# The up projection of the second MLP: twelve column blocks against seven block products per unit, with the sum of stages parked in the output

## What is computed

```python
def reference(**kwargs):
    ...
    x = ...                       # retention over q, k, v: B=2, S=768, 8 heads of 64 -> x is (2, 768, 512)
    x = _moe_ref(x=x, **moe_kwargs)
    return _moe2_ref(x=x, **moe2_kwargs)

def _moe_ref(x, w_theta, w_tok_r, w_tok_i, w_ch):
    theta = x @ w_theta
    zr, zi = x * np.cos(theta), x * np.sin(theta)
    y = np.einsum('ts,bsd->btd', w_tok_r, zr) + np.einsum('ts,bsd->btd', w_tok_i, zi)
    u = x + y
    return u + np.maximum(u @ w_ch, 0.0)

def _moe2_ref(x, w_tok1, w_tok2, w_ch1, w_ch2):
    xt = x.transpose(0, 2, 1)
    h = np.maximum(xt @ w_tok1, 0.0) @ w_tok2          # 768 -> 256 -> 768 tokens
    u = x + h.transpose(0, 2, 1)
    h2 = np.maximum(u @ w_ch1, 0.0) @ w_ch2            # 512 -> 1536 -> 512 channels
    return u + h2
```

## Time and profile before

| what | value |
|---|---|
| time, median of 3 runs | 435.82 us (435.68 to 436.22) |
| the profiled execution: time, span of its instructions | 435.77 us, 434.0 us |
| PE busy, PE weight loads busy | 426.8 us, 388.3 us |
| DVE, ACT, POOL busy | 278.4, 158.3, 85.3 us |
| `tokens_down` on PE | from 228.24 to 244.91 us |
| up projection on PE | from 244.91 to 342.87 us |
| down projection on PE and its last sum | from 342.87 us to the end |

### The profile page before, as it was taken

How to read it: one execution, slowest core, us unless ns; L and a number is a source line. 1 busy time by engine, 2 the same in 40 slices (tenths; PEclk the granted TensorE clock), 3 DMA queues, 4 the chain that set the end, 5 groups by cost and what they waited for, 6 DMA issues and landing times.

```text
span 434.0 us, 6621 instructions
## 1 busy us (share of the span) xinstructions
PE 426.8 (98%) x2748; PEld 388.3 (89%) x2748; DVE 278.4 (64%) x383; ACT 158.3 (36%) x231; POOL 85.3 (20%) x75
## 2 busy tenths in 40 slices
PE   7999999999999999999999999999999999999997
PEld 4778878899999999999889988888888899999997
DVE  3799998799999995234415304525211599999951
ACT  1364564744455456112214311101202443555500
POOL 1322241000300006980005803303000110000000
PEclk9999999999999999999999999999999999999999
DMA  8975797540594102030000000003000468340121
GB/s 301 419 269 198 253 270 146 103 145 2 157 220 159 48 2 97 2 115 31 0 2 0 2 0 0 2 0 142 5 0 2 72 154 171 113 67 26 54 74 73
DMA packets 10478, 42.25 MB, mean 97 GB/s; under 512 B 1104, under 2 KB 3280, under 8 KB 8656
## 3 DMA queue, kind: packets, MB, share of 16 engines
q1 hardware_dynamic: 7344, 26.74, 16.6%
q0 software_dynamic: 2960, 14.94, 15.6%
q10 hardware_dynamic: 144, 0.14, 0.1%
HBM read 38.68 MB, written 3.15 MB: 96 GB/s over the span
## 4 chain that ended last, share of the span: by engine, by line
PE 96%; DVE 2%; DMA 1%; ACT 0%; issue 0%; ACTq 0%; DVEq 0%
PE ps L982 85%; PE ps L999 3%; PE ps L1039 3%; PE ps L1053 2%; PE ps L1130 1%; PE ps L1013 1%; PE ps L1029 1%; DMA qkv_in<-qkv 1%; DVE prob L712 1%; DVE h_ops_c L906 0%; DVE w_sq L696 0%; ACT h_ops_c L657 0%; DVE x_lo L736 0%; DVE res L731 0%; DVE res L942 0%
## 5 line engine op out<-in xcount | busy, mean ns | idle before, releaser
L982 PE MATMUL ps<-u,ch 128*128 128x512 f32 x432 | 98.1, 389 | 0.0
L982 PEld LDWEIGHTS ps<-u,ch 128*128 128x128 f32 x432 | 81.1, 188 | 16.8
L982 PE MATMUL ps<-tw,zs 128*128 128x384 f32 x504 | 88.1, 335 | 0.0
L982 PEld LDWEIGHTS ps<-tw,zs 128*128 128x128 f32 x504 | 87.3, 188 | 0.1
L982 PE MATMUL ps<-h_ops_c,w 128*128 128x384 f32 x312 | 57.0, 335 | 0.2
L982 PEld LDWEIGHTS ps<-h_ops_c,w 128*128 128x128 f32 x312 | 54.2, 188 | 0.8 <-DVE h_ops_c L906 0.8
L899 DVE SCALAR_TENSOR_TENSOR h_a<-ps,h_a 128x512 f32<-128x512 f32 (+1 forms) x16 | 8.9, 558 | 44.3 <-PE ps L982 26.3
L580 ACT ACTIVATE zs<-z 128x768 fp32r<-128x768 f32 x28 | 23.7, 846 | 37.0 <-PE ps L982 37.0
L982 PE MATMUL ps<-ut,w_sq 128*128 128x384 f32 x192 | 35.5, 338 | 0.0
L982 PEld LDWEIGHTS ps<-ut,w_sq 128*128 128x128 f32 x192 | 33.0, 188 | 0.0
L982 PE MATMUL ps<-w_sq,x_hi 128*128 128x512 f32 x96 | 30.7, 401 | 0.7 <-DVE w_sq L696 0.7
(11 more groups left out here) (106 smaller groups left out, 639.0 us busy)
## 6 DMA issues: line engine op xcount, KB each, us to landing
qkv_in<-qkv SPq DMA_DIRECT2D x11, 1024.0 KB, 7.5
raw<-tok POOLq DMA_DIRECT2D x7, 1152.0 KB, 9.0
stage<-weights SPq DMA_DIRECT2D x11, 512.0 KB, 3.4
w_raw<-ch POOLq DMA_DIRECT2D x7, 768.0 KB, 6.8
cols_out<-res SPq DMA_DIRECT2D x16, 192.0 KB, 1.8
raw<-tok SPq DMA_DIRECT2D x6, 384.0 KB, 8.6
w_raw<-ch SPq DMA_DIRECT2D x2, 768.0 KB, 5.3
raw<-tok POOLq DMA_DIRECT2D x3, 384.0 KB, 9.2
```

Of the source, the lines that this page charges most:

```text
L982: mm = pe.matmul(dst, left(l), right(r), start=first and n == 0, stop=last and n == 2, skip_group_check=True)
```

## The change

The up projection too becomes a 2 x 2 block product with seven block products. u of a sequence is cut into channel halves (rows) and token halves (columns); `w_ch1` into its input halves and, for each of six groups phi of 256 hidden channels, two output halves. A unit is (phi, sequence): `UNITS` has 12. Each unit has seven products of 2 k-blocks x 3 passes over 384 tokens, so 504 matmuls of 384 columns stand where 432 of 512 stood. Units go in pairs: product j of unit n, then product j of unit n + 1, then j + 1 (six pairs).

- Of each sequence the seven operands `u_op(b, o)` are made of four blocks and four sums (`sum_u`): seven copies on ACT (`u_high`), seven subtractions (`u_low`). DVE does the low parts of sequence 0 and two of sequence 1, POOL the five others. u_low of the whole u is gone.
- The first product is negated. Products 0, 2, 4 and 6 are added up in one bank (A); after 0, 2 and 4 the bank's running sum is copied or combined: ACT keeps it after products 0 and 2 (`keep_p1`, `keep_p6`) and keeps product 1 of bank B (`keep_p5`), DVE combines after 3, 4 and 5 (`add_p3`, `add_p7`, `add_p2`). A product that adds to a bank waits for the reader of what stood in it: product 2 for `keep_p1`, 3 for `keep_p5`, 4 for `keep_p6`, 6 for `add_p7`.
- POOL's `split_w1` makes, of each 1024-wide piece, 1792 columns of weights: three blocks plain and four with sums (four additions of 256 columns in place). Pieces 0 to 2 are split ahead of the stage, 3 and 4 after pair 1, 5 after pair 3. Stage buffers go from three to two.
- `res` is written to the output after `keep_u2` (2 transfers, "parked"), since its space is wanted for units, and read back into `total` in four transfers during the last pair; `keep_down` adds to `total`, one addition a cell.
- The order of the seven down products, their signs and the loads of `w_ch2` are others; the first load starts once the last piece of `w_ch1` is split, the second only when the whole up projection is done.

```diff
-NSTAGE = 3
+NSTAGE = 2
+UP = 7
+UP_W = (0, 6, 5, 4, 3, 1, 2)
+UP_BANK = (0, 1, 0, 1, 0, 2, 0)
+UP_FRESH = (0, 1, 5)
+UNITS = [(0, 0), (1, 0), (0, 1), (1, 1)] + [(phi, b) for phi in range(2, NPHI) for b in range(B)]
...
+BK_UP = (((1, 2), (4, 5)), ((3, 6), (3, 6)), ((7, 0), (7, 0)))
...
+            for b in range(B):
+                sp.wait_ge(u2_kept, 2 * NK * (b + 1))
+                sp.dma_start(out[b].rearrange("k p s -> p k s"), res[:, b, :, :]).then_inc(spilled[b], 16)
+            load_piece(N_PIECES - 1)
             split_done(sp, N_PIECES - 1)
-            for i in range(2):
-                sp.dma_start(w2_raw[:, i, :], ch2[i]).then_inc(w2_in[i], 16)
+            sp.dma_start(w2_raw(0), ch2[1]).then_inc(w2_in[0], 16)
...
+            sp.wait_ge(up_ready, up_count(len(UNITS) - 1, 3))
+            for b, r in ((0, 0), (1, 1), (1, 0), (0, 1)):
+                sp.dma_start(total[:, b, 2 * r:2 * r + 2, :],
+                             out[b, 2 * r:2 * r + 2].rearrange("k p s -> p k s")).then_inc(back[b][r], 16)
+            sp.wait_ge(up_ready, len(UNITS) * UP)
+            sp.dma_start(w2_raw(1), ch2[0]).then_inc(w2_in[1], 16)
...
+                    if part:
+                        pool.wait_ge(w1_lo, 2 * phi + 1)
+                        pool.tensor_tensor(a11, a11, a21, ALU.add).then_inc(w1_sum, 1)
...
+                        pool.tensor_tensor(a12, a12, a22, ALU.add).then_inc(w1_sum, 1)
...
+                    pool.tensor_scalar(home[:, 0, to], raw1[:, at], 1.0, 1.0, ALU.mult, ALU.mult).then_inc(w1_hi, 1)
...
+                    pool.wait_ge(w1_hi, 2 * phi + part + 1)
+                    pool.tensor_tensor(home[:, 1, to], raw1[:, at], f32(home[:, 0, to]),
+                                       ALU.subtract).then_inc(w1_lo, 1)
...
+            for o in U_PLAIN:
+                u_low(o)
...
             pool.wait_ge(w2_lo, 1)
-            add_w2(0, 2, s2_part)
+            pool.dma_start(w2_raw(0), ch2[3]).then_inc(s1_part, 16)
+            pool.wait_ge(s1_part, 16)
+            add_w2(0, 2, s1_w_in)
...
+            for pair in range(NPAIRS):
+                n = 2 * pair
+                last = pair == NPAIRS - 1
+                if pair == 0:
+                    u_high(0, 4)
+                keep_p1(n)
...
+                keep_p1(n + 1)
+                if pair == 0:
+                    u_high(0, 5)
+                    u_high(0, 6)
...
+                keep_p5(n)
+                keep_p5(n + 1)
...
+            for pair in range(NPAIRS):
+                if pair == 0:
+                    u_low(1, 0)
+                    sum_u(1, 0)
+                    sum_u(1, 1)
+                elif pair == 2:
+                    h_op_low(0, 0)
+                    h_op_low(0, 1)
...
+                add_p3(n)
+                add_p3(n + 1)
+                if pair == 0:
+                    u_low(1, 3)
+                    sum_u(1, 2)
+                for m in second:
+                    second_units(m, 0, 1)
+                add_p7(n)
+                add_p7(n + 1)
...
+                elif j == 2:
+                    pe.wait_ge(p1_kept, n + 1)
+                elif j == 3:
+                    pe.wait_ge(p5_kept, n + 1)
+                elif j == 4:
+                    pe.wait_ge(p6_kept, n + 1)
+                elif j == 6:
+                    pe.wait_ge(sum_22, n + 1)
+                for k in range(2):
+                    mm = three(up_bank(n, j), lambda l: w1_home(phi)[:, l, at:at + P],
+                               lambda r: u_op(b, j)[:, r, k * HS:(k + 1) * HS], j in UP_FRESH and k == 0, k == 1)
```

More of the change, by code:

```diff
@@ L23 @@
 PIECE = 1024
-NSTAGE = 3
+NSTAGE = 2
 NQ = 3
-TILES = 3
 NPHI = NF // 2
@@ new lines, in first_units @@
+            def first_units(n, row, half):
+                to = unit_block(n, row, half)
+                if (row, half) == (1, 0):
+                    act.wait_ge(up_ready, up_count(n, 6))
+                    act.activation(to, up_bank(n, 6), ACT.Relu).then_inc(first_21, 1)
+                else:
+                    added, kept = {(0, 1): (sum_12, first_12), (1, 1): (sum_22, first_22),
+                                   (0, 0): (sum_11, first_11)}[row, half]
+                    act.wait_ge(added, n + 1)
+                    act.activation(to, to, ACT.Relu).then_inc(kept, 1)
@@ new lines, in u_low @@
+            def u_low(b, o):
+                dve.wait_ge(u_hi[b], o + 1)
+                hi, lo, done = f32(u_part(b, o, 0)), u_part(b, o, 1), u_minus_lo if b else u_lo[0]
+                if o in U_MINUS:
+                    dve.scalar_tensor_tensor(out=lo, in0=u_raw(b, o), scalar=-1.0, in1=hi, op0=ALU.mult,
+                                             op1=ALU.subtract).then_inc(done, 1)
+                else:
+                    dve.tensor_tensor(lo, u_raw(b, o), hi, ALU.subtract).then_inc(done, 1)
@@ new lines, in _, with add_p3 @@
+            keep_u2(0, 0, 2)
+            sum_u(0, 0)
+            u_low(0, 0)
+            keep_u2(0, 2, 4)
+            u_low(0, 1)
+            keep_u2(1, 0, 1)
+            sum_u(0, 1)
+            keep_u2(1, 1, 2)
+            u_low(0, 2)
+            keep_u2(1, 2, 3)
+            u_low(0, 3)
+            keep_u2(1, 3, 4)
+            sum_u(0, 2)
+            u_low(0, 4)
+            u_low(0, 5)
+            sum_u(0, 3)
+            u_low(0, 6)
+            def add_p3(n):
+                dve.wait_ge(up_ready, up_count(n, 3))
+                dve.wait_ge(p6_kept, n + 1)
+                to = unit_block(n, 0, 1)
+                dve.tensor_tensor(to, to, up_bank(n, 3), ALU.subtract).then_inc(sum_12, 1)
@@ L948, in _ @@
-            for n in range(len(HIDDEN)):
-                f, tile = HIDDEN[n]
-                if tile != 0:
-                    second_units(n)
-                if tile == 2 and f % 2 and f < 8:
-                    h_op_low(0, f // 2)
-                    h_sums(3, f // 2)
-                if (f, tile) == (10, 2):
-                    w2_low(0)
-            h_op_low(0, 4)
+                if p in (0, 2, 3, 5):
+                    dve.wait_ge(back[b][row], 16)
+                else:
+                    dve.wait_ge(down_kept, {1: 0, 4: 2, 6: 3}[p] * CELLS + i + 1)
```

495 lines of the change are left out of this document (316 added, 179 removed).

## The result

The changed kernel took **441.03 us** (median of four, 439.18 to 443.38) beside 436.02 for the kernel before (four, 435.68 to 437.29): a ratio of 1.011, 95% interval 1.009 to 1.014. It is slower by 5.0 us, and lies above the predicted 434.5 and above the range. Run once more, unaltered and beside experiments 4, 6 and 7, it took 440.57 (ratio 1.010, 1.009 to 1.012).

A forecast was written before the change was run, and what follows sets the result against it. TensorE, busy 426.8 of 434.0 us, was taken to set the end. Terms -10.5 + 4.7 + 1.6 - 0.4 + 3.3 = -1.3 us against the profiled 435.77 gave 434.5 us; range 430.0 to 438.2.

The forecast's parts named there:

- as worked: Whole kernel: the likeliest case, all terms as computed, 433.2 to 436.0 us; chance 0.42.
- Fewer columns: Up projection: 504 matmuls of 384 columns take 87.5 us instead of 97.96, -10.5 us if operands are in time.
- Pair 0, product 3: Up projection: PE waits 1.1 us for `keep_p5(0)`, which stands behind ACT's copy of operand 6.
- Product 6: Pair 0: PE waits 3.6 us for `add_p7(0)` behind DVE's queue and turns with POOL; 1.8 without turns.
- the clock falls: Rival: half rate after the 3.6 us idle before product 6 of pair 0; 25 matmuls make 4.0 us, 438.5; chance 0.12.
- Pair 2: Up projection: DVE and POOL collide, product 6 waits 1.4 us; 0.2 more at ACT's `keep_p1` of pair 3.
- if DVE gets both low parts in one turn: Pair 2, product 6: condition for the 1.4 us wait; 3.4 if POOL comes between, nothing without collision.
- POOL between the low parts: Pair 2: part of the "more turns" rival, +2.0 us; with an even later load 435.5 to 438.5, chance 0.16 together.
- Start of `down`: First product of `down`: its sixth operand is ready before it is wanted, so the old 0.45 us wait goes, -0.4 us.
- The second block of `w_ch2`: Product 1 of `down`: block lands 8.9 us into `down`, +3.3 us; nothing by 5.6, each microsecond later one more.
- landing at 4.9 (no adding transfer in the way): Second `w_ch2` block: lower bound of its landing time in `down`, giving 0 us loss; upper bound 10.9 gives 5.3.
- The rest: Splitting pieces 0 to 2 and parking lie under other work; a late piece 0 has 24 us to spare.

The follow-up runs named there:

- experiment 4: Changed kernel with POOL starting its low parts of sequence 1 only after `sum_u(1, 2)` is done; 438.45 us, ratio 1.0066.
- experiment 6: Changed kernel with GpSimd's adding transfer asked for only after the second `w_ch2` block has landed, SP's load order kept; 435.54 us, ratio 0.9998.
- experiment 7: Changed kernel with loads reordered, adding transfer held back, and DVE and ACT queues reordered in pair 0 and DVE's in pair 2; 424.91 us, ratio 0.9751.
- 1: Changed kernel with the second `w_ch2` block asked for behind one read of the parked sum instead of four; 434.79 us, ratio 0.9987.
- 10: Experiment 7 with the transfers as in the changed kernel: four reads, then the block, adding transfer not held back; 432.58 us, ratio 0.9921.
- experiment 5: Changed kernel with sixteen extra matmuls of 384 columns ahead of PE's wait before product 6 of unit 0; 439.65 us, ratio 1.0091.
- 9: Experiment 7 without the adding transfer's wait for the second `w_ch2` block, all else kept; 425.67 us, ratio 0.9772.
- again: The changed kernel run once more, unaltered, on the chip of experiments 4, 6 and 7; 440.57 us, ratio 1.0104.
- 3: Changed kernel with pair 2's two `h_op_low` behind the `add_p7` on DVE instead of ahead of the `add_p3`; 440.88 us, ratio 1.0114.
- 2: Changed kernel with both `add_p7` of pair 0 ahead of `u_low(1,3)` and `sum_u(1,2)` on DVE; 438.04 us, ratio 1.0053.
- 11: Experiment 7 with DVE's list of pair 2 put back as in the changed kernel; 429.13 us, ratio 0.9849.

## Why the prediction was wrong

Forecast -1.3 us, measured +5.0. The likeliest case, "as worked", did not come; nor did one rival alone, but parts of two, both on the slow side. Step by step:

- **Fewer columns**: -10.5 forecast, -10.4 measured (experiment 7, with 0.2 us of waits in it). Right.
- **Pair 0, product 3**: 1.1 forecast, 1.09, released by ACT's `keep_p5`. Right. **Product 6**: 3.6 forecast, 3.27 of gap; experiment 4 gives 1.75 for the forecast 1.8 without turns. Right in mechanism and size. What followed it was not in the sum.
- **The clock** is the first wrong step: "the clock falls", chance 0.12, 4.0 us at one place. In the traces of the study it was at 0.50 behind product 6 in every execution with that gap left open (five), and three places were struck, not one. The row I leaned on for the main case, a clock of 1.00 at 7 to 9 us, was one execution's: at that very place, behind 1.5 us of idling, experiments 1 and 10 had 0.50. At pair 0 the price is 1.6 us (experiment 5 shows it alone); the 4.0 had 25 matmuls at half rate, there were ten, 320 ns apart. Of the prediction's rule from the Trainium skill, TensorE: Matmul & The Clock Gate, section on the clock gate, that the array drops to half rate after idling and wins it back by work: the traces agree (1.00 before the gap of pair 0, 0.50 behind it, 1.00 again 3.4 us later), and the rival beside it, 438.5, lay nearer to the 441.03 than the main case did.
- **Pair 2**: 1.4 + 0.2 forecast, 2.5 to 2.6 and in five of the eight executions with that gap another 1.6 of half clock. The step "if DVE gets both low parts in one turn" failed; the rival "POOL between the low parts" (+2.0) is what happened, in part. It was mis-sized by two things: POOL's four additions took 0.73 to 0.74 us each where I had 0.63, so that its subtraction ended at 9.96 and not at 9.2 to 9.6; and I counted only POOL's subtractions and additions as takers of turns, while its one-input copy is one too (0.6 to 0.7 us; read from the rows, no experiment takes the copy away alone). The Trainium skill, SBUF — State Buffer, section "SBUF: two separate sides", has the port pair taken for a whole instruction by whoever starts first, against a GpSimd operation that reads SBUF, with no mention of how many inputs that has; the row at 294.00 agrees, and the rule I used in the prediction spoke of DVE's inputs alone.
- **Start of `down`**: -0.4 forecast, -0.7 measured. Right, 0.3 us too small.
- **The second block of `w_ch2`** is the term with the largest error: 3.3 forecast, 6.1 and 6.7 measured, since it landed 11.5 to 11.8 us into `down` and not 8.9. The mechanism was right: "nothing" up to 5.6, "each microsecond later is one more". Landings and losses of product 1 in eleven executions, with the length of the half clock during it ("ch." is the changed kernel):

| execution | 7 | 9 | 1 | 6 | 4 | ch. | 5 | again | 3 | 2 | 10 |
|---|---|---|---|---|---|---|---|---|---|---|---|
| landing, us into `down` | 4.55 | 5.38 | 6.36 | 8.0 | 11.39 | 11.54 | 11.62 | 11.8 | 11.99 | 12.31 | 12.69 |
| loss of product 1, us | 0 | 0 | 0.88 | 2.5 | 6.37 | 6.08 | 6.14 | 6.67 | 7.93 | 6.85 | 7.21 |
| at 0.50, us | 0 | 0 | 0 | 0 | 6.8 | 3.4 | 3.4 | 6.8 | 6.8 | 3.4 | 6.8 |

  Landing less 5.6 gives 0, 0, 0.8, 2.4, 5.8, 5.9, 6.0, 6.2, 6.4, 6.7, 7.1: right to 0.2 us but for 4 and "again" (0.6 and 0.5 more) and 3 (1.5 more), all three with 6.8 us at half clock (10 had as much and fits). What was mis-sized is the DMA work ahead: each read of the parked sum took 2.1 to 2.2 us of all DMA engines where I took 1.9, they began 0.5 later than worked (first packet at 340.3), and a load on POOL's queue was still running then (last packet at 340.9). That the transfer that adds is the largest single one stands: without it the block lands 3.5 us sooner (experiment 6). But the bound "landing at 4.9 (no adding transfer in the way)" was wrong: it landed at 8.0.
- **The rest** (pieces 0 to 2, parking): right; the stage began at 244.77 in the second execution, 244.91 before.
- **The chances**: the prediction adds 0.30, 0.18 and 0.12 up to 0.58; they are 0.60. Nothing hangs on it.

From the forecast -1.3 to the first execution's +3.4 (its late start left out) are 4.7 us: 2.8 the block, 1.6 the clock at pair 0, 1.0 pair 2, less 0.3 each for product 6 and the start of `down`, 0.1 for the stream.

**Where the expected gain went**: -10.6 stream; +1.1 and +3.3 waits for queues in pair 0, +1.6 clock; +2.5 pair 2, +1.6 clock in five of the eight executions; -0.7; +6.1 to +6.7 load. Together +3.4 to +5.5, against a median of +5.0. Two of the parts are shown by putting each back into the mended kernel: loads 7.7 us (10 against 7; 7.2 in the trace), pair 2 4.2 (11 against 7). Pair 0 was not put back alone: 16.1 less 7.7 and 4.2 leaves 4.2 for it, while its losses in the trace are 5.8, so the parts do not quite add up. Why a run's clock falls in pair 2 and not in the next, with the same gap of 2.3 us, stays open; so do the late rise at the start and the early fall in experiments 1 and 10.

## What to carry to other kernels

A stream cut by 10% shows only when each queue is early enough at each product: list, for every wait, what stands ahead of the releaser in its queue, and put the half microsecond that TensorE waits for ahead of the long sums that it does not. Count transfers in the order of issue, other queues' work with them, and ask for what the next stage needs first ahead of what it needs last. Mend all the late places at once: alone, 2 lost part of its gain and 3 all of it at the next place.

## What the runs showed of the hardware

- A gap on PE can cost more than its length. Inside the two stages, losses of the gap alone, and the granted clock behind it: 1.1 us (product 3 of pair 0, wherever it stood) 1.00; 1.75 (experiment 4) and 1.93 (2) 1.00; 2.3 to 2.6 (pairs 2 and 3, nine executions) 1.00 in four, 0.50 in five; 3.3 (pair 0) 0.50 in each of five; 3.2 to 4.5 (product 1 of `down`) 0.50 in each of seven. Early in the program 1.4 to 1.5 us of idling had 0.50 behind it in two executions and 1.00 in the ten others that have a record of the clock there. A stretch of 3.4 us of half clock costs 1.6 us where PE sets the pace, as in pair 0.
- Where DVE sets the pace, at product 1 of `down`, one stretch of half clock cost next to nothing: landing less 5.6 gives the loss to 0.2 us in three executions. With 6.8 us at half clock it was 0.1, 0.5, 0.6 and 1.5 us more.
- A GpSimd copy with one input took 1.55 us instead of 0.83 next to DVE's low part; DVE's sum of two SBUF tiles took 2.56 instead of 0.95 next to GpSimd's subtraction. DVE's operations with one operand in PSUM kept their 0.54 to 0.56.
- Two queues' transfers shared the DMA engines and did not land in the order asked for: SP's four reads, one transfer that adds and the block took 17.5 us at a share of 0.93, and the adding one, asked for at 341.50, landed at 352.46, ahead of two reads asked for at 339.83 and 340.70 (352.72 and 354.59).
